# Second products gathered into runs of eighteen, a lone tile's transposes moved among its products, and GpSimd's store loop nested in turns of three

## The reference

```python
scores = scale * q @ k.T                      # 4 batches, 8 heads, 576 positions, 64 wide
x = (scores * Dmat) @ v                       # decaying causal mask, gives 2304 rows of 512
x = (x @ w_a) * (x @ w_b) @ w_out             # 512 -> 1536 -> 512
logits = x @ w_gate + modality_bias[modality_id]
e_idx = argmax(logits)                        # one of 8 experts for each row
h = maximum(x[mask] @ w1[e], 0)               # 512 -> 1024
out[mask] = gate_w[mask] * (h @ w2[e])        # 1024 -> 512
```

## Time and profile before

| | before |
|---|---|
| median of 3 runs | 784.06 us (783.34 to 785.14) |
| profiled execution | 783.58 us |
| its span, first to last instruction | 781.7 us |
| TensorE busy | 768.6 us, 98% of the span, 4987 products |
| VectorE, ScalarE, GpSimd busy | 55%, 29%, 11% |
| mean granted TensorE clock | 0.998 |

### The profile page before, as it was taken

The page is one execution under the profiler, slowest core; times in us unless marked ns, Lnnn a source line. Parts: engine busy times, 40 slices in busy tenths (PEclk is TensorE's granted clock), DMA queues, the critical chain, the costliest instruction groups (busy, mean ns, idle before and its releaser), DMA issues.

```text
span 781.7 us, 14660 instructions
## 1 busy us (share of the span) xinstructions
PE 768.6 (98%) x4987; PEld 705.3 (90%) x4989; DVE 430.0 (55%) x927; ACT 226.7 (29%) x425; POOL 86.2 (11%) x122
## 2 busy tenths in 40 slices
PE   8999999999999999999999999999999999999995
PEld 5888899999999999999999999999989898998984
DVE  3566543333333488888567888885773532443221
ACT  2333323232233223222234222233202421422110
POOL 2653000000000000000002000000022122030211
PEclk9999999999999999999999999999999999999999
DMA  9998241212121221212453222231215332150000
GB/s 210 226 240 162 55 153 49 81 41 81 43 79 60 62 77 44 81 40 81 125 187 86 76 64 57 81 139 65 82 55 176 136 108 94 41 187 13 29 27 16
DMA packets 101950, 72.45 MB, mean 93 GB/s; under 512 B 46350, under 2 KB 87438, under 8 KB 101776
## 3 DMA queue, kind: packets, MB, share of 16 engines
q1 hardware_dynamic: 82256, 51.44, 24.3%
q0 software_dynamic: 4544, 16.33, 6.3%
q10 hardware_dynamic: 15104, 4.08, 3.1%
HBM read 63.14 MB, written 9.74 MB: 93 GB/s over the span
## 4 chain that ended last, share of the span: by engine, by line
PE 96%; SPq 2%; DMA 1%; issue 0%; DVE 0%; POOL 0%; POOLq 0%; DVEq 0%
PE wide L1388 38%; PE bank L1407 19%; PE bank L2043 14%; PE bank L263 13%; PE bank L724 2%; PE wide L789 2%; PE wide L756 2%; PE bank L779 1%; PE bank L689 1%; PE wide L311 1%; PE bank L694 1%; SPq L501 1%; DMA q_nat<-in_q_dram 1%; PE wide L1419 1%; PE bank L400 1%
## 5 line engine op out<-in xcount | busy, mean ns | idle before, releaser
L1388 PE MATMUL wide<-x,wh 128*128 128x384 f32 x1136 | 289.3, 335 | 0.0
L1388 PEld LDWEIGHTS wide<-x,wh 128*128 128x128 f32 x1136 | 206.9, 188 | 6.1
L1388 PE MATMUL wide<-x,wl 128*128 128x384 f32 x568 | 190.7, 336 | 0.0
L1388 PEld LDWEIGHTS wide<-x,wl 128*128 128x128 f32 x568 | 106.6, 188 | 0.0
L1119 DVE TENSOR_TENSOR hid<-wide,a_sb 128x384 f32<-128x384 f32 x71 | 39.8, 561 | 98.7 <-PE wide L1388 58.1
L994 ACT ACTIVATE hh<-hid 128x384 fp32r<-128x384 f32 x72 | 37.8, 525 | 180.2 <-DVE hid L1119 176.6
L1407 PE MATMUL bank<-wh,hl 128*128 128x512 f32 x216 | 85.5, 396 | 0.0
L1407 PE MATMUL bank<-wl,hh 128*128 128x512 f32 x216 | 85.3, 395 | 0.0
L1407 PE MATMUL bank<-wh,hh 128*128 128x512 f32 x216 | 84.5, 391 | 0.0
L263 PE MATMUL bank<-xTh,expert_whl 128*128 128x384 f32 x320 | 82.4, 336 | 0.0
L2043 PE MATMUL bank<-expert_whl,hTh 128*128 128x512 f32 (+1 forms) x256 | 79.5, 392 | 0.0
(11 more groups left out here) (300 smaller groups left out, 933.1 us busy)
## 6 DMA issues: line engine op xcount, KB each, us to landing
expert_raw<-in_moe_w_dram SPq DMA_DIRECT2D x12, 1024.0 KB, 5.5
raw<-in_moe_w_a_dram SPq DMA_DIRECT2D x36, 256.0 KB, 3.3
raw<-in_moe_w_b_dram SPq DMA_DIRECT2D x36, 256.0 KB, 3.8
raw<-in_moe_w_out_dram SPq DMA_DIRECT2D x36, 256.0 KB, 2.7
q_nat<-in_q_dram SPq DMA_DIRECT2D x16, 256.0 KB, 5.8
k_nat<-in_k_dram SPq DMA_DIRECT2D x28, 128.0 KB, 5.4
x_rows<-x POOLq DMA_DIRECT2D x2, 1548.0 KB, 7.5
v_nat<-in_v_dram ACTq DMA_DIRECT2D x22, 128.0 KB, 5.2
```

Source lines behind the costliest of these rows:

```text
L1388: last = pe.matmul(ps[:, 0:HALF], w[par][m][:, P * t:P * t + P], x[:, g, part, t, cols], start=(k0 == 0), stop=(k0 == 3 * KD - 1))
```

## The change

In 30 of the 36 steps of the feed-forward layer `ab` of both halves is issued first, 48 products, and then `down` of both halves, 18 products. The other six keep the old order: the three "first" steps, "second" of group 2, and "last" of groups 1 and 2. In `rest` the first half's transposes stand behind the first three products of `up_single`'s second half; the second half's stand, when the tile is the last one, behind the first three products of `down_single` and under an `If`; VectorE makes the first low part ahead of the rectifier of its half; the four products without use are gone. GpSimd's loop over units becomes a loop of turns of three, with a test for each turn. One address moves: X2, the region of the experts' transposed rows (xT), from 195,040 to 195,072.

```diff
-    X, ..., X2 = (0, 73728, ..., 188544, 195040)
+    X, ..., X2 = (0, 73728, ..., 188544, 195072)
...
                 ab(Fi, Fp, par, 0, g, False)
+                if where in ("middle", "gates") or where == "last" and g == 0 or opening and g < GROUPS - 1:
+
+                    ab(Fi, Fp, par, 1, g, False)
+                    for half in range(2):
+                        down(Fi - 1, 1 - par, half, opening, ending, claim)
+                    return
...
-        with pool.Fori(1, UNITS) as u:
-            with pool.If(u * OPEN < total):
-                body(u)
+        with pool.Fori(0, STORE_TURNS) as turn:
+
+            with pool.If((turn * 3 + 1) * OPEN < total):
+                with pool.Fori(0, 3) as i:
+                    with pool.If((turn * 3 + 1 + i) * OPEN < total):
+                        body(turn * 3 + 1 + i)
...
         def rest(u):
             t = u * OPEN
+            transposed_low(t, range(1))
             hidden_low(t)
-            transposed_low(t)
+            transposed_low(t, range(1, 2))
...
-            for half in range(2):
-                up_single(0, loads, half)
-            hidden_transposed(t)
+            up_single(0, loads, 0)
+            up_single(0, loads, 1, lambda: half_transposed(t, 0))
             with pe.If(t + 1 < total):
+
+                half_transposed(t, 1)
                 second = of_plan(pe, t + 1, 0, 0, RUNS - 1)
                 for half in range(2):
                     up_single(1, second, half)

-            for _ in range(BRIDGE):
-                pe.matmul(ex.ps_x[1][:, :], ones[:, :], ones[:, :].unsqueeze(1).broadcast_to([P, 4, P]),
-                          start=True, stop=True)
-            down_single(t, 0, loads)
+            def alone():
+                with pe.If(t + 1 >= total):
+                    half_transposed(t, 1)
+            down_single(t, 0, loads, alone)
```

More of the change, by code:

```diff
@@ L52 @@
 SECOND_TURNS = -(-(-(-N // WIDE)) // 3)
+STORE_TURNS = -(-(UNITS - 1) // 3)
 MOD = 2
@@ L134 @@
     X, RAW, W, HID, X2_ODD, X2T, GATE, FREE, SMALL, X2 = (
-        0, 73728, 86016, 110592, 129024, 141408, 153696, 170080, 188544, 195040)
+        0, 73728, 86016, 110592, 129024, 141408, 153696, 170080, 188544, 195072)
     Z, LOW, HIDDEN = 131072, 147520, 155648
@@ L1965, in hidden_low, with transposed_low @@
             dve.tensor_scalar(hid[1][:, :], ps_h[1][:, :], 0.0, None, ALU.max).then_inc(s_hd, 1)
-        def transposed_low(t):
-            for half in range(2):
+        def transposed_low(t, halves=range(2)):
+            for half in halves:
                 dve.wait_ge(s_hth, 2 * t + 1 + half)
@@ L2101, in unit, with up_single @@
                 down_tile(u, False, loads, i)
-        def up_single(i, loads, half):
+        def up_single(i, loads, half, behind_first=None):
             pe.wait_ge(s_wl, QUARTERS * loads + half + 1)
@@ L2107, in up_single, with half_transposed, down_single @@
             at = slice(P * i, P * i + P)
-            products(ps_h[half][:, :], [(high[:, n, at], low[:, n, at]) for n in range(KD)],
-                     weights(loads, half), True, True).then_inc(s_h, 1)
+            left, right = [(high[:, n, at], low[:, n, at]) for n in range(KD)], weights(loads, half)
+            products(ps_h[half][:, :], left[:1], right[:1], True, False)
+            if behind_first is not None:
+                behind_first()
+            products(ps_h[half][:, :], left[1:], right[1:], False, True).then_inc(s_h, 1)
+        def half_transposed(t, half):
+            pe.wait_ge(s_hd if half else s_ha, t + 1)
+            pe.sem_inc(s_passed, 1)
+            for n in range(KF // 2):
+                last = pe.transpose(ps_h[2 + half][:, P * n:P * n + P], hid[half][:, P * n:P * n + P], ident)
+            last.then_inc(s_ht, 1)
         def hidden_transposed(t):
             for half in range(2):
[L2113 to L2119, removed]
+                half_transposed(t, half)
+        def down_single(t, i, loads, behind_first=None):
             bank_free(t, i)
@@ L2124, in down_single @@
                 pe.wait_ge(s_htl, 2 * t + half + 1)
-                last = products(ps_y[i % 2][:, :], [(hTh[half][:, P * n:P * n + P], hTl[half][:, P * n:P * n + P])
-                                                    for n in range(KD)], weights(loads, 2 + half), half == 0, half == 1)
+                left = [(hTh[half][:, P * n:P * n + P], hTl[half][:, P * n:P * n + P]) for n in range(KD)]
+                right = weights(loads, 2 + half)
+                products(ps_y[i % 2][:, :], left[:1], right[:1], half == 0, False)
+                if half == 0 and behind_first is not None:
+                    behind_first()
+                last = products(ps_y[i % 2][:, :], left[1:], right[1:], False, half == 1)
             last.then_inc(s_ymm, 1)
```

1 line of the change is left out of this document (removed).

## The result

The changed kernel takes **780.42 us** in the median of 11 runs (779.94 to 783.58); the kernel before, run beside it, 784.3 (783.23 to 787.78, 11 runs). The ratio is 0.9957, with a 95% interval of 0.9945 to 0.997. The profiled execution took 780.41, its span is 778.6 against 781.7. The prediction said 780.3 and 3.5 us less; the two spans differ by 3.1, the two medians by 3.9.

What follows compares the result with a forecast made beforehand. TensorE, busy for 98% of the span, was taken as the bound. Steps 2.4 plus end 1.1 give 3.5 us: 783.58 to 780.1, up to 780.6 with the median's offset, stated as 780.3; range 779.0 to 782.0.

Steps and rivals of the forecast that it cites:

- Runs of eighteen: Feed-forward steps: a run of 48 and one of 18 products save 0.08 us in each of 30 steps, 2.4 us.
- VectorE's cover: Dotting steps: VectorE's `product` still comes in time for the second half's b products; cost nothing, cover perhaps down to 0.1 us.
- a wait ahead of the second half's b products: Sign that the forecast is wrong: TensorE waiting there in groups 1 and 2 of the feed-forward layer.
- The lone tile: In `rest` near the kernel's end: the new order starts the last product 0.84 us sooner; omitting useless products adds nothing.
- The address: Moving X2 speeds the lone tile's 24 first products, 0.1 us taken, 0.14 at most; nothing for the units' 384-column products.
- The store loop: Kernel's end: fewer skipped units let GpSimd's DRAIN start sooner, 0.6 us taken, bounds 0 and 0.9.
- The end together: Kernel's end: GpSimd would end 1.5 us sooner, but TensorE becomes last, so 1.1 us gained, bounds 0.3 and 1.9.
- the rival: A far branch on TensorE near the end: one more dear branch costs 0.75 us, giving 780.9 to 781.4; chance 0.15.
- the pace doesn't depend on the neighbours: Rival for the feed-forward steps: they keep 12.53 us and only the end gains, 782.5 us; chance 0.10.
- VectorE decides the dotting steps: Rival: a VectorE cycle of 13.0 us makes TensorE wait in 16 steps, 786.7 us; chance 0.03.

Runs made afterwards that it cites:

- The second comparison: The unaltered changed kernel measured again, beside one with a weight split moved earlier: 780.97 us against 783.32 for the kernel before, ratio 0.9966.
- the kernel with equal columns: The changed kernel with 384 in place of 512 columns in every second product but the one opening each bank, so leaving out work: 763.51 us.
- the loop alone: The kernel before with only the store loop in turns of three: 785.87 us in one run, whose clock fell for a while.
- the lone tile alone: The kernel before with only the new `rest`, without the four useless products, with old steps, address and store loop: 782.47 us, one run.
- the steps alone: The kernel before with only the runs of eighteen in the feed-forward steps: 782.3 us in the median against 783.58, ratio 0.9983.

## Why the prediction was right

The time is within 0.2 us of the forecast, and that is in part luck. The parts below add up to a gain of 2.9 us and not 3.5, errors of both signs met, and 784.06 less 2.9 would be 781.2. The second comparison gave 780.97 and a gain of 2.35.

- *Runs of eighteen*, 2.4 us: mis-sized. The saving is 0.067 a step, 2.0 us in all, inside the bounds (1.9 to 2.8). I had put 0.07 for the case in which a run of 48 that is entered from a run of 512 columns "costs once more the excess", and took 0.08 because the 96 products that follow 72 in the experts showed hardly any. That row was the wrong neighbour: it hides the excess only at the old address, and shows the full 26 ns at the new one. The runs of 24 were the right neighbour, and the kernel with equal columns shows that their excess comes with the change of the column count.
- *VectorE's cover*, "cost: nothing": the step that failed. In the dotting steps it held: I read a cycle of at most 12.58 us, it is 12.23 to 12.43, and the lag shrinks where I let it grow. By the starts in the changed kernel, `product` of the first half begins 0.48 us after that half's matmuls have ended, at most, in the second group, and in the third this falls from 1.31 to 0.65. The bound was near all the same: the one that came 1.87 late cost 0.51, so a wait begins at about 1.36, where I had 1.4. But I had looked at the dot products alone. Step two of the last group gives VectorE 4.49 us of splits right ahead of a first half in the new order, and that cost 0.51 us, which moving one of the splits gave back. The sign of error that I had named, "a wait ahead of the second half's b products", is what was seen.
- *The lone tile*, 0.84: measured 0.81 alone. The products without use, which I put at nothing, gave 0.09 when they alone were omitted. The second transposes wait 0.32 us where I had 0.48.
- *The address*, 0.1 of at most 0.14: 0.09 in the tile. But for the 384-column products of the units I wrote "nothing there", and they lose 0.10, so the term is nothing on the whole. My reason, that their pace equals that of the feed-forward layer, was read at the old address and says nothing of the new one.
- *The store loop*, 0.6: 0.60, and 0.61 with the loop alone. By the two lengths of the DRAIN the limit is the end of the store instruction.
- *The end together*, 1.1: too low, it is 1.5, as the sum of its parts. I expected TensorE's DRAIN at 780.2 to 780.5, and so last. With the 1.62 us by which all came sooner it stands at 779.7: the branch took 0.44 and not 0.96. GpSimd stays last by 0.26 us. With the lone tile alone the branch took 1.24 and TensorE was last. So this term hangs on a branch whose price neither the diff nor the trace of before gives; the rival named it, but expected it to get dearer, and in this build it got cheaper.
- The rivals: that the pace doesn't depend on the neighbours is refuted by the steps alone; that VectorE decides the dotting steps, by its cycle of at most 12.43 us.

Together 2.0 - 0.5 - 0.1 + 0.9 + 0.6 = 2.9, and 0.2 of chance ahead of the feed-forward layer makes the 3.1 of the spans, for the 3.5 foretold.

## What to carry to other kernels

Where TensorE is full, put products of equal column count side by side. Take the excess from runs of the same operands at the same addresses: a row elsewhere showed 5 ns where the full excess was 26, and a shift of 32 bytes brought the 26 back. An address that helps one stage is to be read in every stage that uses the operand. When runs are drawn together, list for every step, not for the common one, what the evacuating engines have in their queues: the two places that cost time here (0.5 and 1.6 us) were a single step with weight splits and a last step whose products had covered a weight split. Below 1 us at the end of a kernel, read each engine's own end; which is last can hang on one branch.

## What the runs showed of the hardware

- In the feed-forward layer a change of the column count makes the next products slower by up to 12 ns each, over nine of 512 or six of 384 columns, 41 and 26 ns in all; changes that follow each other quickly cost less each (4 pairs 0.148 us a step, 2 pairs 0.133, 1 pair 0.067). With equal column counts it is nothing.
- In the experts' units the same excess of 26 ns is 5 ns when the moving operand lies 32 bytes lower.
- A stationary operand moved up by 32 bytes changes a product of 512 columns from 233 to 227 ns in the lone tile.
- In three of the twelve profiled executions of the full computation TensorE's granted clock falls to 0.50, its lower level of 1.2 GHz, for 6.8 us from 550.6, 552.1 or 552.8 us on, between the two layers. From the end of the feed-forward layer to the lone tile these take 217.0 to 217.2 us, the others 213.8 to 214.0. The kernel with the store loop alone; start and end of the stretch, its length, busy us and instructions of PE, PEld, DVE, ACT and POOL, then the granted clock, the share of DMA and GB/s:

```profile
540.00:552.00 12.00, 12.00 (x92) 11.05 (x90) 7.55 (x14) 5.46 (x10) 0.00 (x0) 1.00 0.01 1
552.00:554.00 2.00, 2.00 (x13) 2.00 (x12) 0.56 (x1) 0.00 (x0) 0.00 (x0) 0.70 0.00 0
554.00:558.00 4.00, 4.00 (x16) 4.00 (x16) 1.87 (x11) 0.73 (x2) 0.00 (x0) 0.50 0.00 0
```

In the 10 us before the fall TensorE made transposes, products of 8 columns for the gates and a few of 384 columns, without a pause, in the executions that kept the clock as in those that lost it. In the stretch at the lower level products of 384 columns follow at 320 ns and not 173. What decides between the two the traces don't show.
